# Routed experts behind top-32 attention: small sums, one division, slot names and weight halves moved between engines

## Time and profile before

| | us |
|---|---|
| median of 3 runs | 909.51 (908.22 to 910.8) |
| profiled execution, its own time | 909.91 |
| profiled execution, span from first to last instruction | 908.2 |
| TensorE busy | 865.3 (95%) |
| VectorE busy | 547.8 (60%) |
| ScalarE busy | 341.6 (38%) |
| GpSimd busy | 296.5 (33%) |
| mean granted clock of TensorE | 0.968 |

### The profile page before, as it was taken

One profiled execution on the slowest core, in us unless ns is written; L12 is line 12 of the kernel. 1 busy time (PEld: TensorE's weight loads), 2 busy tenths in 40 slices (PEclk: granted clock), 3 DMA queues, 4 the chain that ended last, 5 costly groups with the idle time before them and its releaser, 6 DMA issues.

```text
span 908.2 us, 13642 instructions
## 1 busy us (share of the span) xinstructions
PE 865.3 (95%) x4921; PEld 724.3 (80%) x4921; DVE 547.8 (60%) x1086; ACT 341.6 (38%) x726; POOL 296.5 (33%) x243
## 2 busy tenths in 40 slices
PE   7699999967999999899999999999999999999998
PEld 5588888854766666767778889889898999899886
DVE  5999999999999999844472633333141422342121
ACT  5455555544664775423562513222030311122010
POOL 7876677648686679302010300000000000000000
PEclk9599999987999999989999999999999999999999
DMA  9320000051363563037182510202002200000001
GB/s 205 99 93 21 16 13 13 13 168 53 119 231 112 202 210 116 13 118 278 48 334 106 206 64 1 93 1 93 1 1 92 92 0 0 0 0 0 35 22 47
DMA packets 49394, 75.60 MB, mean 83 GB/s; under 512 B 24624, under 2 KB 24624, under 8 KB 49328
## 3 DMA queue, kind: packets, MB, share of 16 engines
q1 hardware_dynamic: 43088, 60.62, 19.8%
q0 software_dynamic: 4160, 13.63, 4.9%
q10 hardware_dynamic: 2080, 0.52, 0.3%
HBM read 63.49 MB, written 11.27 MB: 82 GB/s over the span
## 4 chain that ended last, share of the span: by engine, by line
PE 59%; DVE 21%; POOL 9%; issue 8%; ACT 2%; DMA 0%; DVEq 0%; SPq 0%; POOLq 0%; ACTq 0%
PE bank L1514 17%; PE bank L1516 17%; PE bank L1515 17%; DVE work L1116 9%; DVE top L1121 7%; POOL att L670 5%; DVE top L1107 3%; POOL att L673 2%; PE bank L1509 2%; PE bank L1670 2%; PE bank L1575 1%; PE bank L1693 1%; PE bank L1654 1%; POOL xs_raw L691 1%; ACT w2h L899 1%
## 5 line engine op out<-in xcount | busy, mean ns | idle before, releaser
L1121 DVE MAX8 top<-work 128x8 f32<-128x576 f32 x216 | 152.5, 744 | 0.0
L670 POOL TENSOR_SCALAR att<-sc,top 128x576 f32<-128x576 f32 x70 | 120.8, 1726 | 81.9 <-DVE top L1121 81.7
L1514 PE MATMUL bank<-xT,w1h 128*128 128x384 f32 x384 | 128.7, 335 | 1.5 <-DVE w1l L1348 1.5
L1451 DVE SCALAR_TENSOR_TENSOR hT<-bank,hT 128x384 fp32r<-128x384 f32 x96 | 52.8, 557 | 126.1 <-ACT hT L1019 125.6
L1516 PE MATMUL bank<-xT,w1h 128*128 128x384 f32 x384 | 128.4, 334 | 0.0
L1515 PE MATMUL bank<-xT,w1l 128*128 128x384 f32 x384 | 128.3, 334 | 0.0
L1019 ACT ACTIVATE hT<-bank 128x384 fp32r<-128x384 f32 x96 | 46.9, 492 | 195.4 <-PE bank L1516 195.3
L1516 PE MATMUL bank<-w2l,hT 128*128 128x512 f32 x288 | 112.2, 390 | 0.0
L1515 PE MATMUL bank<-w2h,hT 128*128 128x512 f32 x288 | 112.2, 390 | 0.0
L1514 PE MATMUL bank<-w2h,hT 128*128 128x512 f32 x288 | 112.1, 389 | 0.0
L1116 DVE MATCH_REPLACE8 work<-top,work 128x576 f32<-128x576 f32 x144 | 106.5, 746 | 0.0
(11 more groups left out here) (274 smaller groups left out, 1439.7 us busy)
## 6 DMA issues: line engine op xcount, KB each, us to landing
w_raw<-in_moe_w_dram SPq DMA_DIRECT2D x92, 512.0 KB, 6.2
q_raw<-in_q_dram SPq DMA_DIRECT2D x18, 128.0 KB, 3.0
v_one<-in_v_dram POOLq DMA_DIRECT2D x18, 128.0 KB, 5.0
out_dram<-x_tok SPq DMA_DIRECT2D x9, 256.0 KB, 2.0
y_dram<-zero POOLq DMA_DIRECT2D x2, 1024.0 KB, 7.1
w_early<-in_moe_w_dram SPq DMA_DIRECT2D x4, 512.0 KB, 8.8
y_dram<-b_ys POOLq DMA_DIRECT2D x7, 256.0 KB, 3.7
k_raw<-in_k_dram SPq DMA_DIRECT2D x6, 256.0 KB, 4.6
```

The lines of the kernel that those rows point to most:

```text
L670: nc.gpsimd.tensor_scalar(att[:, g % ATR, :], sc[:, g % RING, :], top8[:, g % RING, 3, 7:8], None, ALU.is_ge).then_inc(keep_made, 1)
L1121: nxt = nc.vector.max(out=top8[:, g % RING, i + 1, :], in_=work[:, j, :])
L1451: nc.vector.scalar_tensor_tensor(out=hTl(b)[:, f, :], in0=bank[:, HB + f % 4, 0:BW], scalar=0.0, in1=f32(hTh(b)[:, f, :]), op0=ALU.max, op ...
L1514: nc.tensor.matmul(dst, high_lhs, high_rhs, start=start, stop=False)
```

## The change

- **Small divisions' sums on GpSimd.** For the tiles 0 to 7 the 1e-9 is added by GpSimd (`safe_sums`, after mask 8t+11) into a new tensor den_safe; VectorE's reciprocal waits for it (den_made). The last tile stays as it was.
- **Tile 2's multiplication on GpSimd.** ON_POOL now holds 2.
- **The first group's slot names and gates.** L1317 and L1318 of GA move to GpSimd, ahead of the first gather; the three gate steps of GA move on VectorE from pair 36 to behind the last mask.
- **Marks summed.** GpSimd forms running sums of GB's one-hot marks (hot_sums, five additions and a copy, after its last mask and ahead of a guarded branch); TensorE's six products with ones become one, which waits for them.
- **Unread products moved.** See the last hunks: fewer behind the steps 72 to 75, some ahead of att_times_v, one and two in the last logits and ranks, 7 in place of 13 before slot 0.
- **w2 of the first expert.** SP waits for slot 0's rows before it loads the parts 2 and 3; ScalarE and VectorE split part 2 before, and part 3 between, the hidden rows of slot 0.
- **Last slot.** GpSimd splits part 0 of w1 ahead of its last store, VectorE waits for it and does the others.

```diff
-        ON_POOL = (0, 1, 3, 4, 5, 6)
+        ON_POOL = (0, 1, 2, 3, 4, 5, 6)
...
                     sp.wait_ge(a_d, SPREAD)
+                    sp.wait_ge(slot_loaded[0], 16)
                     first_down((2, 3))
...
+            def safe_sums(t):
+                pool.wait_ge(av_copied, t * H + H)
+                if t >= 1:
+                    pool.wait_ge(rden_made, t)
+                nc.gpsimd.tensor_scalar(den_safe[:, :].rearrange("p (h o) -> p h o", o=1), av[:, t % 2, :, D:W], 1e-9, None, ALU.add).then_inc(den_made, 1)
+
             def divided(t):
-                pool.wait_ge(norm_step, 2 * t + 2)
+                pool.wait_ge(rden_made, t + 1)
...
             def beside():
                 yield from clock.until(TOKENS_AT)
+                pool.wait_ge(by_slot_made, 2)
+                nc.gpsimd.tensor_scalar(GA.by_slot_i[:, 0, :], GA.by_slot[:, 0, :], -1.0, None, ALU.add).then_inc(GA.table_made, 1)
+                nc.gpsimd.tensor_copy(GA.by_slot_i[:, 1, :], GA.by_slot[:, 1, :]).then_inc(GA.table_made, 1)
                 pool.wait_ge(x_kept, 16 * TB)
...
                 mask(g)
+                if g % H == 3 and 0 <= g // H - 1 < T - 1:
+                    safe_sums(g // H - 1)
                 if g % H == 4 and g // H - 1 in ON_POOL:
                     divided(g // H - 1)
...
+            pool.wait_ge(GB.hot_made, 1)
+            for t in range(GB.tiles - 1):
+                if t >= 1:
+                    pool.wait_ge(sums_made, t)
+                nc.gpsimd.tensor_tensor(hot_sums[:, t + 1, :], hot_sums[:, t, :], GB.onehot[:, t, :], ALU.add).then_inc(sums_made, 1)
+            pool.wait_ge(sums_made, GB.tiles - 1)
+            nc.gpsimd.tensor_copy(hot_sums[:, GB.tiles, :], hot_sums[:, GB.tiles - 1, :]).then_inc(sums_made, 1)
             with pool.If(guarded(pool, GA, SPREAD)):
...
             def last_stored(slots):
+                pool.wait_ge(w1_high, ke * DC + 1)
+                nc.gpsimd.tensor_tensor(w1l[:, 0:1, :], w1_raw[:, 0:1, :], f32(w1h[:, 0:1, :]), ALU.subtract).then_inc(w1_split, 1)
                 store_slot(slots - 1)
...
                     nc.scalar.activation(b_hs[:, i * 512:(i + 1) * 512], bank[:, HB + i, :], ACT.Relu).then_inc(slot_relu, 1)
+                    if i == 0 and s == 0:
+                        split_high(0, w2_raw, w2h, w2_loaded, w2_high, (2,))
...
                     nc.scalar.activation(b_hsTh[:, 4 * i:4 * i + 4, :], four(bank[:, HTB + i, :]), ACT.Copy).then_inc(slot_hT_high, 1)
-                if s == 0:
-                    split_high(0, w2_raw, w2h, w2_loaded, w2_high, (2, 3))
+                    if i == 0 and s == 0:
+                        split_high(0, w2_raw, w2h, w2_loaded, w2_high, (3,))
...
                 def first():
+                    if t < T - 1:
+                        return
...
                 def second():
-                    dve.wait_ge(norm_step, k + 1)
                     if t >= 1:
                         dve.wait_ge(x_ready, t)
+                    if t < T - 1:
+                        dve.wait_ge(den_made, t + 1)
+                        nc.vector.reciprocal(rden[:, :], den_safe[:, :]).then_inc(rden_made, 1)
+                        return
+                    dve.wait_ge(norm_step, k + 1)
                     nc.vector.reciprocal(rden[:, heads], den[:, heads]).then_inc(norm_step, 1)
...
             turn_experts()
+            for _ in gates(GA):
+                pass
...
                 for i in range(2):
+                    if i == 0 and s == 0:
+                        split_low(0, w2_raw, w2h, w2l, w2_high, w2_split, (2,))
...
+                    if i == 0 and s == 0:
+                        split_low(0, w2_raw, w2h, w2l, w2_high, w2_split, (3,))
                     if i == 0:
                         slot_xT_low(s + 1)
-                if s == 0:
-                    split_low(0, w2_raw, w2h, w2l, w2_high, w2_split, (2, 3))
...
             def last_slot(s):
-                split_low(ke, w1_raw, w1h, w1l, w1_high, w1_split, (0, 1))
+                dve.wait_ge(w1_split, ke * DC + 1 + BASE)
+                split_low(ke, w1_raw, w1h, w1l, w1_high, w1_split, (1,))
...
                 nc.tensor.transpose(bank[:, TBK, 0:P], x_cur[:, (DC - 1) * P:DC * P], ident[:, :]).then_inc(x_rest_made, 1)
+                fill(MB + 2, 1)
...
+                else:
+                    pe.wait_ge(sums_made, n)
+                    last = nc.tensor.matmul(rows[:, 0:(n + 1) * E], ones[:, :], hot_sums[:, :, :].rearrange("p t e -> p (t e)"), start=False, stop=False)
                 last.then_inc(g.rank_made, 1)
...
+                if HEADS < p < AV_END:
+                    fill(MB + 2, (0, 2, 2, 4, 1)[p - HEADS])
                 if 0 <= p - AV_LAG < HEADS:
                     att_times_v(p - AV_LAG)
                 if logits_at(p) == T - 2:
                     x_logits(T - 2)
-                if HEADS <= p < AV_END - 1:
-                    fill(MB + 2, 4 if p < HEADS + 3 else 7)
+                if HEADS <= p < HEADS + 3:
+                    fill(MB + 2, 2)
...
             ranks(GB)
+            fill(MB + 2, 2)
             last_ranks()
...
-            fill(MB, 13)
+            fill(MB, 7)
```

More of the change, by code:

```diff
@@ L93, in attention_and_experts @@
         rden = consts.take("rden", [P, H])
+        den_safe = consts.take("den_safe", [P, H])
         before = consts.take("before", [P, P])
@@ L153, in attention_and_experts @@
         hot_last = consts.take("hot_last", [P, E])
+        hot_sums = consts.take("hot_sums", [P, GB.tiles + 1, E])
         routing_tensors(GA, consts)
@@ L283, in attention_and_experts @@
         c_cols = sem("c_cols")
+        sums_made = sem("sums_made")
         v_ones = sem("v_ones")
@@ L311, in attention_and_experts @@
         norm_step = sem("norm_step")
+        den_made = sem("den_made")
+        rden_made = sem("rden_made")
+        by_slot_made = sem("by_slot_made")
         x_ready = sem("x_ready")
@@ L649, in _ @@
             nc.gpsimd.memset(GB.onehot[:, :, :], 0.0).then_inc(c_cols, 1)
-            pool.wait_ge(c_cols, 9)
+            nc.gpsimd.memset(hot_sums[:, :, :], 0.0).then_inc(c_cols, 1)
+            pool.wait_ge(c_cols, 10)
             nc.gpsimd.tensor_scalar(ecol_less[:, :], ecol_i[:, :], -E, None, ALU.add).then_inc(c_cols, 1)
@@ L750, in _ @@
             slots = pool.value_load(GB.table_i[0:1, 0, E:E + 1], min_val=1, max_val=GB.slots)
+            ke = pool.value_load(GB.table_i[0:1, 1, E:E + 1], min_val=1, max_val=E)
             def last_stored(slots):
+                pool.wait_ge(w1_high, ke * DC + 1)
+                nc.gpsimd.tensor_tensor(w1l[:, 0:1, :], w1_raw[:, 0:1, :], f32(w1h[:, 0:1, :]), ALU.subtract).then_inc(w1_split, 1)
                 store_slot(slots - 1)
@@ L1144, in third @@
                         return
-                    dve.wait_ge(norm_step, k + 2)
+                    if t < T - 1:
+                        dve.wait_ge(rden_made, t + 1)
+                    else:
+                        dve.wait_ge(norm_step, k + 2)
                     if t >= 1:
@@ L1172, in pick @@
                 dve.wait_ge(turn_read, turn_use["lg", g.first + b - 1])
-                dve.wait_ge(c_cols, 15)
+                dve.wait_ge(c_cols, 16)
                 step(nc.vector.tensor_tensor(lg, lg, bias_t[:, tiles, :], ALU.add))
@@ L1312, in place @@
                 settle()
-                go(g, nc.vector.tensor_copy(g.by_slot[:, 1, 0:1], g.by_slot[:, 0, 0:1]))
-                go(g, nc.vector.tensor_tensor(g.by_slot[:, 1, 1:s], g.by_slot[:, 0, 1:s], g.by_slot[:, 0, 0:s - 1], ALU.subtract))
-                yield
-                settle()
-                nc.vector.tensor_scalar(g.by_slot_i[:, 0, :], g.by_slot[:, 0, :], -1.0, None, ALU.add).then_inc(g.table_made, 1)
-                nc.vector.tensor_copy(g.by_slot_i[:, 1, :], g.by_slot[:, 1, :]).then_inc(g.table_made, 1)
-                if g is GB:
+                if g is GA:
+                    nc.vector.tensor_copy(g.by_slot[:, 1, 0:1], g.by_slot[:, 0, 0:1]).then_inc(by_slot_made, 1)
+                    nc.vector.tensor_tensor(g.by_slot[:, 1, 1:s], g.by_slot[:, 0, 1:s], g.by_slot[:, 0, 0:s - 1], ALU.subtract).then_inc(by_slot_made, 1)
+                    yield
+                else:
+                    go(g, nc.vector.tensor_copy(g.by_slot[:, 1, 0:1], g.by_slot[:, 0, 0:1]))
+                    go(g, nc.vector.tensor_tensor(g.by_slot[:, 1, 1:s], g.by_slot[:, 0, 1:s], g.by_slot[:, 0, 0:s - 1], ALU.subtract))
+                    settle()
+                    nc.vector.tensor_scalar(g.by_slot_i[:, 0, :], g.by_slot[:, 0, :], -1.0, None, ALU.add).then_inc(g.table_made, 1)
+                    nc.vector.tensor_copy(g.by_slot_i[:, 1, :], g.by_slot[:, 1, :]).then_inc(g.table_made, 1)
                     go(g, nc.vector.tensor_scalar(g.kth_expert[:, :], g.kth_expert[:, :], first_less[:, :], None, ALU.add))
@@ L1329, in place, with gates, settle @@
                     token_numbers()
-                yield
```

(20 more changed lines are left out.)

1 line of the change is left out of this document (removed).

## The result

The changed kernel takes 911.86 us (median of 20 runs, 910.39 to 916.06); the kernel before took 909.35 beside it (20 runs, 907.23 to 911.47). The ratio is 1.0032, interval 1.0022 to 1.0042: slower by 0.3%, where 904.6 us was predicted. The profiled execution took 913.42 us (span 911.7) for 909.91 (908.2).

What follows compares the result with a forecast made beforehand. VectorE was taken to set the pace up to the last threshold, TensorE in the slots. Slot 0's rows -3.2, w2 -1.2 and last slot -0.9 made -5.3: 909.9 to 904.6 us; range 899.4 to 909.5.

Steps and rivals of the forecast that it cites:

- Tile 3's 4.4 us: VectorE's reciprocal at tile 3 waits 4.4 us for GpSimd's add, which stands behind the gather and mask 35.
- tile 7's 2.2: VectorE's reciprocal at tile 7 waits 2.2 us for GpSimd's add, behind a weight split and mask 67.
- the logits' 0.9: VectorE's pick at tile 2 waits 0.9 us for logits, since GpSimd's division makes x_cur later.
- the rival in which they don't form: VectorE's waits for GpSimd don't form, last masks -4.5 instead of +3.0, 899.4 us; chance 0.17.
- the rival of dear small GpSimd instructions: The eight adds and six sums cost 1.5 us each instead of 0.3: +12.4, so 917 us; chance 0.08.
- the rival of eaten gains: Half clock through the tail (+0.9), w2 part 2 late (+2), last slot gives nothing (+0.9): 908.4 us; chance 0.23.
- VectorE up to the last masks: Removals and new waits on VectorE through tile 7 together make its last two masks +3.0 us late.
- The sums themselves: Adds removed from VectorE: 1.2 us gained for tiles 0 to 6, 1.4 for tile 7's.
- The turn of slot 0's rows: -3.2: TensorE turns slot 0's rows 3.2 us earlier, the middle between -4.0 at full clock and -2.3 at half.
- The marks' sums: -1.7: In the ranks, one pair of products replaces twelve on TensorE, GpSimd's sums being hidden: -1.7 us.
- Slot 0's w2: Splitting part 2 ahead of slot 0's hidden rows removes TensorE's 1.59 us wait for w2l: -1.2 us.
- The last slot: GpSimd splits w1l part 0 earlier, shortening TensorE's 1.49 us wait: -0.9 us (0 and -1.5).

Runs made afterwards that it cites:

- experiment 1: Changed kernel with GpSimd's small sums one mask earlier (behind mask 8t+10 instead of 8t+11): 904.09 us, ratio 0.9916.
- experiment 7: Changed kernel with the small divisions' sums back on VectorE for all tiles, no padding: 909.64 us, ratio 0.9975.
- experiment 11: Changed kernel with the small divisions' sums on VectorE and four more unread products at the start: 904.96 us, ratio 0.9943.
- experiment 12: Changed kernel with GpSimd's sums one mask earlier and four more unread products at the start, tile 2's product staying on GpSimd: 901.82 us, ratio 0.9907.
- experiment 10: Changed kernel with one more unread product at the start (8 for 7), 4 instructions: 912.38 us, ratio 1.0034.
- experiment 5: Changed kernel with sums one mask earlier, tile 2's product on VectorE and four more unread products at the start (16 instructions): 898.53 us, ratio 0.9856.
- experiment 14: Changed kernel with sums one mask earlier, tile 2's product on VectorE, four more unread products at the start, repeated on another chip: 899.39 us, ratio 0.9883.
- experiment 6: Changed kernel with four more unread products at the start and no other edit: 906.99 us, ratio 0.9948.
- experiment 3: Changed kernel with GpSimd's sums one mask earlier and tile 2's product back on VectorE, no padding: 903.29 us, ratio 0.9915.
- experiment 15: Changed kernel with sums one mask earlier, four more unread products at the start, tile 2's product on GpSimd, repeated on another chip: 899.99 us, ratio 0.9895.
- experiment 4: Changed kernel with the unread products back where they stood before, thirteen before slot 0 again: 913.89 us, ratio 1.0030.
- experiment 8: Changed kernel with sums one mask earlier, tile 2's product on VectorE and the marks' sums back on TensorE, no padding: 901.49 us, ratio 0.9888.
- experiment 9: Kernel before the change with four more unread products at the start, no other edit: 909.09 us, ratio 0.9995.
- experiment 13: Changed kernel, sums one mask earlier, tile 2's product and last slot's first w1 part on VectorE, four more unread products at the start: 899.52 us, ratio 0.9890.
- experiment 2: Changed kernel with tile 2's multiplication back on VectorE: 911.69 us, ratio 1.0004.

## Why the prediction was wrong

**The waits: right.** Tile 3's 4.4 us (predicted 4.4), tile 7's 2.2 (2.2) and the logits' 0.9 (0.9) came to a tenth. Experiment 1 shows that the first two cost all of their length, and the rival in which they don't form was refuted. So was the rival of dear small GpSimd instructions (0.26 us for a moved sum). Of the rival of eaten gains two parts came true, the half clock in the tail and the last slot, but not the late part 2 of w2.

**VectorE up to the last masks: right in kind, 0.7 to 1.4 off.** +3.7 for +3.0, and +4.4 from the first threshold on. What failed is that the sum took the short instructions' lengths of before (0.16 for the bias) as constants while it moved them by a microsecond against GpSimd's products. Two of them landed inside a product and cost about 1.0 and 0.9 more; another of the same block took 0.65 less (L1219, 0.16 for 0.81) and one 0.3 more, so the block cost 1.5 more in all, and 3.0 + 1.5 is the 4.4 within a tenth. The page SBUF — State Buffer, section two separate sides, of the Trainium skill was quoted for the lock, and the trace agrees again (1.17 and 1.34 us, until the product's end); it was applied to the instructions that were removed, not to those that were shifted. The sums themselves were priced about right: 1.2 for seven and 1.4 for the eighth, 2.6 us, where experiments 7 and 11 beside 1 and 12 give 2.8 and 2.7.

**"The turn of slot 0's rows: -3.2" is the step that failed**; it came out at +5.3. Its issue gap of 1.47 was copied from before, as if it belonged to the place in the program, and measured 4.71. Of the 8.5 us between the two, 3.9 were lost by the token numbers: 2.1 late (401.23 for 399.11), where the middle of the two clock levels had them 1.8 early. TensorE came to them at 399.96, where the sum had 395.2 at full clock and 397.0 at half. Nearly all of that was lost ahead of last_ranks, which began at 394.53 for the sum's 390.4: 0.8 by the late masks and 3.3 between them and last_ranks, in the half clock from 385 to 398.7, while the sum had let the two levels differ only behind last_ranks. How long the half clock lasts differs from one execution to the next: with 13.7 us of it (the changed kernel and experiment 10) the token numbers followed the first of the last two masks after 19.1 us, in the other twelve kernels that sum the marks on GpSimd, at 3.4 or 6.8 us of it, after 15.4 to 17.3, and experiments 5 and 14, one and the same kernel, took 15.6 and 17.0. No run separates its cause. The other 4.6 came behind the token numbers: the stop's 3.3 and some 1.3 for seven products at half clock.

Without the stop the changed kernel has a ratio of 0.9948 (experiment 6), and 904.6 over 909.5 is 0.9946. That the forecast's number comes back is partly luck. The stop and the clock behind it are 4.6 us by the rows, 0.5%, but the ratio moved by 0.8%; the padded profile also had VectorE 1.0 us earlier from the start and a shorter half clock, while the last slot and the collisions at tile 2 stayed worse than the sum had them. In the other pairs with and without the stop the ratio differs by 0.3% (7 and 11), 0.3 to 0.6% (3 and 5 or 14) and only 0.1 to 0.2% (1 and 12 or 15). Each pair ran on two chips, and what is left between 0.1 and 0.8% no run separates: that the stop forms and goes is shown by the rows, what it is worth in time only roughly.

By a rule of the Trainium skill this could have been asked beforehand. The page Runtime: NRT & Kernel Launch, section Instruction fetch mechanics, says that instructions come in blocks of 256 (16 KiB), that crossing a block is mostly hidden, and that a taken branch whose target lies outside the fetched window stalls until its block is there. The trace agrees with the stall (3.3 to 3.9 us at the branch, and packets of 0.02 MB on the instruction queue). It does not agree with "mostly hidden" for the block behind the branch target: here that one cost 3.3 us. That it had not been fetched yet when the sequencer came to its edge is the reading that fits experiments 4, 5, 6, 8, 9 and 10; the edge itself shows in no view.

**The marks' sums: -1.7 predicted, not confirmed by a time.** On GpSimd they are hidden as said (0.26 each). But putting them back on TensorE (experiment 8) made the kernel no slower than experiment 3, since it also moved the code and the stop went. Experiment 5 on the same chip, where the stop is gone too, is 0.3% faster (898.53 for 901.49 us), with intervals that touch. In the two profiles the token numbers follow the last masks 0.9 us sooner with the sums on GpSimd (15.55 for 16.43), at about half the term.

**Slot 0's w2: right** (-1.4 for -1.2). **The last slot: wrong in kind.** GpSimd did its part as timed (from 505.67, behind ScalarE, 2.40 long), but the wait of 1.49 that it was to shorten was never for w1l. It belongs to the branch: in all four profiles read for it TensorE goes on 0.6 us after the branch's end, and in experiment 13 the other engine for the part changes nothing. The 0.3 is about the branch's 3.5 us for 3.9. The prediction had taken the releaser in brackets at its word although w1l had been ready 0.8 us before TensorE went on.

## What to carry to other kernels

Before a small instruction is moved to another engine, find the one there that it will stand behind: one mask earlier was worth 6.75 us at the last masks in experiment 1, for an instruction of 0.26 us. And a short instruction that a change shifts in time can land behind one of another engine and take seven times as long. Where a kernel takes a branch, look at the sequencer's rows behind it; if a second stop of some 3 us follows within a few instructions, some idle instructions ahead may move it away (sixteen did here, four did not), and an edit to that engine's stream can bring it back. A comparison of two versions across such a branch measures the code's position along with the edit, so a padded control belongs to it.

## What was not expected of the hardware

The branch over the rare slots held TensorE's sequencer for 3.3 to 5.4 us (5.4 in experiment 2), and the one behind the last slot for 3.3 to 3.9; the branch behind the slot before took 0.08. A second stop of 2.0 to about 4 us followed within some instructions in the seven kernels whose stream ahead of the branch was the changed kernel's, three instructions shorter or four longer, and in none where sixteen or more had been added, put back or never removed; five removed products were enough. Instructions of 24 columns took 0.16 us alone and up to 1.34 us when they met a GpSimd product. One-operand sums of eight columns on VectorE took 0.14 us where GpSimd waited, 0.37 until the end of a mask comparison on GpSimd, and 1.47 until the end of a weight split. One and the same kernel had ratios of 0.9856 and 0.9883 on two chips (experiments 5 and 14), with overlapping intervals.
